# An attention and mixture-of-experts kernel on one core: two casts ahead of an exponential, an output copy one step later, and the first gates spread by TensorE

## The reference

```python
# attention: batch 4, heads 8, seq S=576, head_dim D=64
scores = scale * np.matmul(q, k.transpose(0, 1, 3, 2))
cum = np.cumsum(np.log(np.clip(f, 0.0001, 1.0)), axis=-1)
scores = np.where(causal, -1e9, scores + cum[..., :, None] - cum[..., None, :])
attn = np.exp(scores - scores.max(-1, keepdims=True))
x = matmul(attn / (attn.sum(-1, keepdims=True) + 1e-9), v)   # to (2304 tokens, 512)
# feed-forward, 512 -> 2048 -> 512
h = x @ w_in
g = np.where(h >= 1, h, np.where(h <= -1, 0, (h + 1) ** 2 / 4))
y = g @ w_out
# mixture of 8 experts, the best one for each token
yn = y / (norm(y) + 1e-6);  en = expert_emb / (norm(expert_emb) + 1e-6)
idx = argmax(yn @ en.T / tau)
out = gate * (relu(y @ w1[idx]) @ w2[idx])                  # 512 -> 1024 -> 512
```

## Time and profile before

| | |
|---|---|
| median of 3 runs | 849.34 us (848.88 to 849.74) |
| the profiled execution | 848.67 us |
| its span, first to last instruction | 846.5 us |
| busy in the span: TensorE, its weight loads | 831.4 us (98%), 778.9 us (92%) |
| VectorE, ScalarE, GpSimd | 410.8, 392.9, 353.0 us |
| mean granted TensorE clock | 0.996 |

### The profile page before, as it was taken

One profiled execution on the slowest core, in us unless ns is written; L12 is line 12 of the kernel. 1 busy time (PEld: TensorE's weight loads), 2 busy tenths in 40 slices (PEclk: granted clock), 3 DMA queues, 4 the chain that ended last, 5 costly groups with the idle time before them and its releaser, 6 DMA issues.

```text
span 846.5 us, 13803 instructions
## 1 busy us (share of the span) xinstructions
PE 831.4 (98%) x5018; PEld 778.9 (92%) x5019; DVE 410.8 (49%) x1002; ACT 392.9 (46%) x916; POOL 353.0 (42%) x366
## 2 busy tenths in 40 slices
PE   7999999999999999999999999999999999999996
PEld 5888888889999999999999999999998998998985
DVE  5888888887555454454444444455534110110200
ACT  6777877876665444534544534433332121111121
POOL 5776778856665020211111202074311692010295
PEclk9999999999999999999999999999999999999999
DMA  7577988962000310301211033252222354304041
GB/s 223 189 246 232 288 264 285 291 207 57 29 1 2 102 57 29 104 29 56 75 56 57 1 103 106 75 163 63 76 101 87 120 167 125 87 37 125 26 138 42
DMA packets 70941, 95.62 MB, mean 113 GB/s; under 512 B 7174, under 2 KB 47110, under 8 KB 70864
## 3 DMA queue, kind: packets, MB, share of 16 engines
q1 hardware_dynamic: 62688, 80.33, 31.3%
q10 hardware_dynamic: 6416, 9.59, 3.2%
q0 software_dynamic: 1760, 4.72, 1.5%
HBM read 70.87 MB, written 24.27 MB: 112 GB/s over the span
## 4 chain that ended last, share of the span: by engine, by line
PE 96%; DVE 2%; DMA 1%; issue 1%; ACT 0%; POOL 0%; POOLq 0%; DVEq 0%; SPq 0%; ACTq 0%
PE psum L1523 25%; PE psum L1525 24%; PE psum L1524 24%; PE psum L1494 6%; PE psum L1450 5%; PE psum L1477 5%; PE psum L1455 2%; PE psum L1447 1%; PE psum L1431 1%; DVE pr L1112 1%; PE psum L1606 1%; PE psum L1590 0%; PE psum L1591 0%; DMA c<-cum_d 0%; DVE ptl L1134 0%
## 5 line engine op out<-in xcount | busy, mean ns | idle before, releaser
L1523 PE MATMUL psum<-xh,winh 128*128 128x384 f32 x384 | 129.0, 336 | 0.0
L1523 PE MATMUL psum<-gh,wouth 128*128 128x384 f32 x384 | 128.3, 334 | 0.2 <-issue 0.2
L1525 PE MATMUL psum<-xh,winl 128*128 128x384 f32 x384 | 128.4, 334 | 0.0
L1524 PE MATMUL psum<-xl,winh 128*128 128x384 f32 x384 | 128.3, 334 | 0.0
L1525 PE MATMUL psum<-gh,woutl 128*128 128x384 f32 x384 | 128.3, 334 | 0.0
L1524 PE MATMUL psum<-gl,wouth 128*128 128x384 f32 x384 | 128.3, 334 | 0.0
L898 ACT ACTIVATE hpos<-psum,minus 128x384 f32<-128x384 f32 x96 | 55.9, 582 | 142.3 <-DVE hclip L1160 142.1
L1165 DVE TENSOR_TENSOR g<-hpos,hsq 128x384 f32<-128x384 f32 x96 | 64.5, 672 | 109.2 <-ACT hsq L900 109.2
L691 POOL TENSOR_TENSOR xst<-xst 128x384 f32<-128x384 f32 x24 | 24.7, 1031 | 178.4 <-DMA xst<-rinv_d 178.2
L1270 DVE SCALAR_TENSOR_TENSOR hl<-psum,hh 128x384 fp32r<-128x384 f32 x48 | 26.8, 558 | 139.4 <-ACT hh L954 139.4
L1169 DVE TENSOR_TENSOR gl<-g,gh 128x384 fp32r<-128x384 f32 x96 | 64.1, 668 | 61.0 <-ACT gh L931 61.0
(11 more groups left out here) (233 smaller groups left out, 1871.6 us busy)
## 6 DMA issues: line engine op xcount, KB each, us to landing
praw<-moe_w SPq DMA_DIRECT2D x48, 256.0 KB, 2.8
qraw<-q SPq DMA_DIRECT2D x15, 448.0 KB, 4.5
vraw<-vk SPq DMA_DIRECT2D x16, 320.0 KB, 3.8
xh<-yh_d SPq DMA_DIRECT2D x20, 256.0 KB, 4.2
xl<-yl_d SPq DMA_DIRECT2D x20, 256.0 KB, 4.6
kraw<-k SPq DMA_DIRECT2D x16, 288.0 KB, 3.8
xa_d<-xo SPq DMA_DIRECT2D x16, 288.0 KB, 4.0
xb_d<-xo SPq DMA_DIRECT2D x16, 288.0 KB, 4.5
```

The lines of the kernel that those rows point to most:

```text
L1523: nc.tensor.matmul(psum_at, ah, bh, start=start, stop=False)
L1524: nc.tensor.matmul(psum_at, ah, bl, start=False, stop=False)
L1525: return nc.tensor.matmul(psum_at, al, bh, start=False, stop=stop)
```

## The change

It has five parts.

1. `CASTS_FIRST` becomes (5, 7). At the ScalarE step whose preceding block is 7 the casts `high(p, 4)` and `high(p, 5)` now stand before `exp(n + 2)`, as they did already for block 5.
2. `copy_early(p)` moves from the step of block 8 to that of block 0 of the next pair, behind `high(p, 6)` and `high(p, 7)`.
3. `low(p, 0)` moves one step later, behind the next `masked`.
4. The gates of pair 0: GpSimd makes a 2 x 128 matrix `spread` of ones and zeros; TensorE multiplies it with two rows of `fc` after the warming matmuls, into the banks `PX` and `PY`; ScalarE copies that to `c8`. The two loads for pair 0 go, SP's wait for `cum_out` moves behind four other loads' issues, and GpSimd's zeroing of parts of `pr` also waits for the spread.
5. The embedding's normalization moves from step -4 to 0, its transposes from step 0 to 3, its cast from 1 to 4 and its low part from 2 to 5.

```diff
--- before.py
+++ after.py
@@ -78,7 +78,7 @@
     POOL_HIGH = 4
     EARLY = 2
-    CASTS_FIRST = 5
+    CASTS_FIRST = (5, 7)
     RAW = 2
@@ -213,6 +213,9 @@
         rsum = sb("rsum", [P, 2, NB], F32, actx)
         rden = sb("rden", [P, 2, NB], F32, actx)
+        spread = rturn[0:2, 0, :]
         emb, emb_sq, norm_e = xo[0:E, 1, 0, 0:DM], xo[0:E, 1, 1, 0:DM], xo[0:E, 1, 0, DM:DM + 3]
         fr = pr[0:HEADS, 0:S]
@@ -267,6 +270,7 @@
         f_in = sem("f_in"); clip_ok = sem("clip_ok"); log_ok = sem("log_ok"); cum_ok = sem("cum_ok")
+        spread_ok = sem("spread_ok"); c_spread = sem("c_spread"); c_first = sem("c_first")
         cum_done = sem("cum_done"); cum_out = sem("cum_out")
         passed = sem("passed")
         counts_ok = sem("counts_ok")
@@ -426,8 +430,7 @@
             def load_c(p):
                 if p >= 2:
                     sp.wait_ge(lowest, NB * (p - 1))
-
-                for h in range(2 if p else 1):
+                for h in range(2):
                     sp.dma_start(c8[h * D:(h + 1) * D, p % 2, :],
                                  cum_d[2 * p + h:2 * p + h + 1, :].to_broadcast([D, S])).then_inc(c_in[p % 2], 16)
@@ -468,13 +471,12 @@
             sp.dma_start(tau_sb[:], tau.unsqueeze(0).to_broadcast([P, 1])).then_inc(emb_in, 16)
             sp.wait_ge(cum_ok, 1)
             sp.dma_start(cum_d, fc).then_inc(cum_out, 16)
-            sp.wait_ge(cum_out, 16)
-            load_c(0)
             load_k(1)
             load_v(0)
             sp.dma_start(xst[:].rearrange("p a c -> p (a c)")[:, 0:(NB - RAW) * P],
                          q[1, :, RAW:NB, :].rearrange("p i r -> p (i r)")).then_inc(q1_in, 16)
             load_first(1)
+            sp.wait_ge(cum_out, 16)
             load_c(1)
             load_k(2)
             load_q(2)
@@ -656,7 +658,15 @@
             nc.gpsimd.tensor_copy(mask_b[D:P, :], mask_w[D:P, D:P]).then_inc(const_ok, 1)
             pool.wait_ge(const_ok, 2)
             nc.gpsimd.memset(rinv[:], 0.0).then_inc(zero_ok, 1)
+            nc.gpsimd.memset(spread, 1.0).then_inc(spread_ok, 1)
+            pool.wait_ge(spread_ok, 1)
+            nc.gpsimd.affine_select(out=spread, in_=spread, compare_op=ALU.is_ge, fill=0.0, base=0,
+                                    pattern=[[1, P]], channel_multiplier=-D).then_inc(spread_ok, 1)
+            pool.wait_ge(spread_ok, 2)
+            nc.gpsimd.affine_select(out=spread, in_=spread, compare_op=ALU.is_ge, fill=0.0, base=D - 1,
+                                    pattern=[[-1, P]], channel_multiplier=D).then_inc(spread_ok, 1)
             pool.wait_ge(cum_out, 16)
+            pool.wait_ge(c_spread, 1)
             for i in range(0, NB, 2):
                 x = nc.gpsimd.memset(pr[:, at_tile(i) + keys(i):at_tile(i) + keys(i) + D], 0.0)
             x.then_inc(zero_ok, 1)
@@ -850,8 +860,8 @@
             nc.scalar.copy(kh[:, 0, :], kraw[:]).then_inc(k_h, 1)
             act.wait_ge(q_in, 16)
             nc.scalar.copy(qh[:, 0], qraw[:]).then_inc(q_h, 1)
-            act.wait_ge(cum_out, 16)
-            act.dma_start(c8[D:P, 0, :], cum_d[1:2, :].to_broadcast([D, S])).then_inc(c_in[0], 16)
+            act.wait_ge(c_spread, 1)
+            nc.scalar.copy(c8[:, 0, :].rearrange("p (a c) -> p a c", a=2), psum[:, PX:PY + 1, 0:S // 2]).then_inc(c_first, 1)
             act.wait_ge(esq_ok, 1)
             nc.scalar.activation(norm_e[:, 1:2], norm_e[:, 0:1], ACT.Sqrt).then_inc(eroot_ok, 1)
@@ -902,21 +912,21 @@
             for n in range(-AHEAD, STEPS + 1):
                 p, i = tile_of(n - 1)
-                if i != CASTS_FIRST and 0 <= n + 2 < STEPS:
+                if i not in CASTS_FIRST and 0 <= n + 2 < STEPS:
                     exp(n + 2)
                 if 0 <= n - 1 < STEPS:
                     for k in fills_of(i):
                         high(p, k)
-                if i == CASTS_FIRST and 0 <= n + 2 < STEPS:
+                if i in CASTS_FIRST and 0 <= n + 2 < STEPS:
                     exp(n + 2)
                 p, i = tile_of(n)
-                if i == 8 and 0 <= p < PAIRS:
-                    copy_early(p)
+                if i == 0 and 0 <= p - 1 < PAIRS:
+                    copy_early(p - 1)
                 if p - 1 in X_LOADED and i == 1:
                     split_x(X_LOADED.index(p - 1))
                 if n == STEPS:
                     rise(0)
-                if n == 1:
+                if n == 4:
                     act.wait_ge(en_turned, 1)
                     nc.scalar.copy(ent[:, :, 0:E], psum[:, PY, 0:KD * E].rearrange(
                         "p (k e) -> p k e", e=E)).then_inc(ent_h, 1)
@@ -1092,8 +1102,10 @@
             def masked(n):
                 p, i = tile_of(n)
                 w = keys(i)
-                if i == 0:
-                    dve.wait_ge(c_in[p % 2], 32 * (p // 2 + 1))
+                if n == 0:
+                    dve.wait_ge(c_first, 1)
+                elif i == 0:
+                    dve.wait_ge(c_in[p % 2], 32 * ((p + 1) // 2))
                 if n == 0:
                     dve.wait_ge(zero_ok, 2)
                 dve.wait_ge(scored, n + 1)
@@ -1178,7 +1190,8 @@
                     masked(n + 4)
                 p, i = tile_of(n - 1)
                 if 0 <= n - 1 < STEPS:
-                    for k in fills_of(i):
+                    for k in fills_of(i) if i not in (1, 2) else fills_of(i - 1):
                         low(p, k)
                     if i == 8 and p >= 1:
                         copy_turned(p - 1)
@@ -1207,7 +1220,7 @@
                 if n == STEPS + 4:
                     add(1)
                     low_g(1)
-                if n == -AHEAD:
+                if n == 0:
                     step(nc.vector.reciprocal(tau_inv[:], tau_sb[:]))
                     dve.wait_ge(eroot_ok, 1)
                     step(nc.vector.tensor_scalar_max(norm_e[:, 1:2], norm_e[:, 1:2], 1.0e-30))
@@ -1217,7 +1230,7 @@
                     step(nc.vector.tensor_scalar(norm_e[:, 2:3], norm_e[:, 2:3], 0.5, 1.0e-6, ALU.mult, ALU.add))
                     step(nc.vector.reciprocal(norm_e[:, 1:2], norm_e[:, 2:3]))
                     nc.vector.tensor_scalar(emb, emb, norm_e[:, 1:2], None, ALU.mult).then_inc(en_ok, 1)
-                if n == 2:
+                if n == 5:
                     dve.wait_ge(ent_h, 1)
                     nc.vector.tensor_tensor(ent[:, :, E:2 * E], psum[:, PY, 0:KD * E].rearrange(
                         "p (k e) -> p k e", e=E), ent[:, :, 0:E].bitcast(F32), ALU.subtract).then_inc(ent_ok, 1)
@@ -1419,6 +1432,13 @@
             for n in range(WARM):
                 nc.tensor.matmul(psum[:, PY, :].rearrange("p (a b) -> p a b", a=4), ident_b[:],
                                  ident_b[:].unsqueeze(1).to_broadcast([P, 4, P]), start=True, stop=True)
+            pe.wait_ge(cum_ok, 1)
+            pe.wait_ge(spread_ok, 3)
+            for j in range(2):
+                x = nc.tensor.matmul(psum[:, PX + j, 0:S // 2], spread, fc[0:2, j * (S // 2):(j + 1) * (S // 2)],
+                                     start=True, stop=True)
+            x.then_inc(c_spread, 1)
             MASK_LATER = (4,)
@@ -1551,7 +1571,7 @@
                         turn(p, k)
                 if n == STEPS - 1:
                     up_block(1)
-                if n == 0:
+                if n == 3:
                     pe.wait_ge(en_ok, 1)
                     for m in range(KD):
                         x = nc.tensor.transpose(psum[:, PY, m * E:(m + 1) * E], emb[:, m * P:(m + 1) * P],
```

## The result

The changed kernel takes 841.74 us (median of 4 runs, 840.90 to 842.73). The kernel before took 849.54 beside it (4 runs, 848.88 to 850.49). The ratio is 0.9908, 95% interval 0.9891 to 0.9925. The profiled execution has a span of 839.7 us against 846.5.

The account below looks back on a forecast made before the run. TensorE was taken to bound attention, with two waits of 7.4 us in the pairs. Gains of 6.8 (waits) and 0.8 (start) less 0.45 (end) made 7.15 us: 842.2 us, range 840 to 846 with rivals.

Parts of the forecast that it names:

- the likeliest case: Whole kernel: two TensorE waits in the pairs mostly go and the start gains; 842.2 us, chance 0.58.
- start: First pair: gates spread by TensorE and embedding moved later bring masked(8) near 18.6 instead of 19.38 us; gain 0.8 us.
- pairs 1 to 14 and the last pair: Attention's pairs: TensorE's waits of 7.4 us go, less 0.3 staying and 0.3 in pair 2; gain 6.8 us.
- end: Last pair: the moved output copy delays ScalarE's chain to the first GpSimd splits, near 208 us; loss 0.45 us.
- (a): Middle pairs: casts before exp(1) start low(4) 0.38 earlier, removing the fifth transpose's wait; 0.28 in 13 pairs, 4.3 us in all.
- rival C: Pairs, slower: ScalarE's queue behind the two casts ends later, so turn(0) waits over 0.5 us; about 851 us, chance 0.03.
- (b): Middle pairs: low(0) behind masked(6) removes score(8)'s wait; 0.16 in 10 pairs plus 1.5 in three long stops, 3.1 us.
- (c): Middle pairs: the output's 0.61 us copy moves into ScalarE's 1.14 us wait for masked(4) and costs nothing.
- The holds: Pair 2: GpSimd's instruction holds VectorE's small denominator add; about 1 us of the hold stays, costing 0.3 us.
- the signs that the prediction named as wrong: VectorE L1211 to L1219 over 0.6 us, clock 0.5 after 12 us, L1477 waiting for exp, wait at 208 over 1 us.
- Rival A: Start: GpSimd's splits hold the embedding's VectorE instructions, making the start 1.5 to 3 us worse; 844.5 us, chance 0.22.
- The clock: Start: no TensorE gap, so 2.4 GHz throughout; a fall for some 3.3 us would cost 1.6 us.

Follow-up runs that it names:

- experiment 1: The kernel before with only parts 1 to 3 of the change (casts first, output copy later, low(0) later), old start kept: 842.09 us, ratio 0.9918.
- experiment 3: The changed kernel with part 1 alone taken back, casts 4 and 5 behind exp(1) again: 844.04 us, ratio 0.9951.
- Experiment 4: The changed kernel with part 3 alone taken back, low(0) between masked(5) and masked(6) again: 843.10 us, ratio 0.9938.
- experiment 5: The changed kernel with part 2 alone taken back, the output's copy at the step of block 8 again: 845.27 us, ratio 0.9957.
- experiment 7: The changed kernel with ScalarE's square root moved ahead of its wait for the spread gates: 842.54 us, ratio 0.9923.
- experiment 6: The changed kernel without the denominator's add of 1e-9, the reciprocal taken of the sum itself: 841.17 us, ratio 0.9911.
- Experiment 9: The changed kernel without the denominator's add, with 10 warming matmuls before the spread and 4 after instead of 22 before: 839.37 us, in two groups, ratio 0.9912.
- experiment 2: The changed kernel with parts 1 to 3 taken back, leaving the new start alone: 849.79 us, ratio 1.0008.
- experiment 11: The kernel before, unchanged, in a second single profiled execution: 848.95 us.
- Experiment 8: The kernel before with six more warming matmuls behind score(2), result unused, to fill TensorE's idle gap: 848.81 us, ratio 0.9998.
- experiment 10: The kernel before with only parts 1 to 3 of the change, old start kept, and without the denominator's add: 841.82 us, ratio 0.9915.

## Why the prediction was right, and where its terms were off

**The total and the likeliest case held.** 841.74 against 842.2. By the profiled spans the terms stand like this: start 1.37 measured, 0.8 predicted; pairs 1 to 14 and the last pair together 4.88 + 0.19 + 0.42 = 5.49, 6.8 predicted (the 0.42 is the end's loss, which lies in the last stretch); end -0.42, -0.45 predicted; and 0.3 in the unchanged rest. Two misses of size cancelled in part, which is luck. By medians the steady parts alone won 6.6 us (experiment 1 against the runs of before beside it); the sum without the start had 6.8 - 0.45 = 6.35. The 0.8 of the start has no run behind it.

**Casts first (a): right.** Predicted 0.28 a pair, experiment 3 gives 0.31, with the stop back in the list 13 times. The mechanism, cast to low(4) to the bank of the fifth transpose, is shown by the 0.38 that VectorE idles less and by that experiment. The delayed exponential cost nothing in ordinary pairs, as forecast, so rival C was not met.

**Low(0) behind masked(6) (b): the wait went, but either of two moves removes it.** The prediction credits 0.16 in ten pairs to this move. Experiment 4 leaves it out and the 0.14 doesn't come back; experiment 3 leaves out the earlier casts and keeps this move, and it doesn't come back either. So the mechanism works, and beside (a) it is worth nothing in an ordinary pair. The wait does come back, as 0.40 us and more of idling, in pairs with an x split, where the prediction put 1.5 us in three stops. Taking it back costs 1.4 us of median, at the limit of what the two intervals tell apart.

**The copy one step later (c): mis-sized.** "It costs nothing" was true of its new place within the pairs, but the old place had a price that no sum of mine had: 0.24 a pair and 3.5 us of median (experiment 5). Before, it seems to have lain in the shadow of the wait that (a) removes: with the copy and low(0) moved and the casts late, ordinary pairs take 11.38 for 11.55 (experiment 3), which is little more than low(0)'s 0.14. No run moves the copy alone. Each ordinary pair won 0.48, the forecast was 0.44; it came out because (c), at nothing in the sum, was part of the change.

**The holds: the step that was off by most.** The prediction kept one in pair 2, for 0.3 us beyond its base. Pair 2 was worse than that (11.90, against 11.07 without it), and there were three more in pairs 11 to 13, where GpSimd's split of v, no longer waiting for a late TensorE, begins 0.97, 1.82 and 1.08 us behind the pair's first score in place of 0.33 and falls over the add. The new wait at the transposes for an exponential, 1.7 us in four stops, is one of the signs that the prediction named as wrong; all four lie in pairs 2, 12 and 13.

What they cost together is known less well. From the third to the last pair it is 146.67 to 146.70 us in both executions of the changed kernel and in experiment 7, and 144.83 and 145.75 without the add (experiments 6 and 9): 0.9 to 1.9. Pair 2's share is 0.8. In the others the late gates of pair 12 and the splits of x are mixed in, and experiment 7 has the whole time without their holds.

Both starts can have pair 2's hold. There GpSimd waits for v's transfer. Its split begins 1.58 to 1.68 us behind the pair's first score in the first execution of before, both of the changed kernel and experiments 3 and 7, and the add takes 1.43 to 1.53. It begins at 0.69 and 0.73 in experiments 2 and 4 (new start) and at 2.15 and 2.39 in 11 and 1 (old start), and the add takes 0.35 to 0.60; experiment 5 lies between, at 1.25 and 1.10. So it hangs on the moment at which v lands, measured from the pair's start. Which of the change's parts sets that moment was not isolated.

**The start: order right, value not visible.** Step by step: first score predicted 10.7, measured 10.41; gates 11.4 and 11.15; masked(4) 14.6 and 14.20; masked(8) 18.6 and 18.00; clock 1.00 throughout, as predicted. Rival A was wrong: the seven embedding instructions ran from 12.58 to 14.26 without a hold, the last in 0.47, its length of the earlier trace rows, though GpSimd was splitting nearly all the while. For the last of them that was no hard test: the split before it had only 0.16 us to go, and the next one began 0.24 us into it. Exp(0) starts 1.30 behind the start of the table load; the drain that the Trainium skill (ScalarE: Activation LUTs, What ACT_TABLE_LOAD costs) puts behind such a load did not show.

But the time of experiment 2 says that this start is worth nothing by itself. The traces give three reasons. Experiment 8, which fills the gap and wins nothing either, bears on the first and the third; no run isolates one. First, the base was one execution in which the clock fell; experiment 11 had no fall and started its third pair 0.59 earlier. Its second pair starts at 17.87, and at 17.14 in experiment 1, also with the old start; with the new one it is 17.43 in the changed kernel and 17.94 in experiment 2. Second, the new start hangs on the end of the warming matmuls, and so on when the clock rises: first scores stand at 10.29 to 11.64 us over the eight profiled executions with it and all 22 of them; the old start waited until 11.7 for the gates and hid this. Third, in the old order of the pairs the earlier start was paid back as waits for masked(6) (2.1 us before; 4.0, 3.1 and 4.1 in experiments 2, 8 and 11). There VectorE's split of x, ahead of masked(5), is held by GpSimd to about 0.95 us in seven, five and seven pairs, and was in three before. The prediction had seen these stops but not what makes them long. I did not make an experiment that moves GpSimd's work alone.

**The clock.** In the profiled execution of before it fell, with a mean of 0.996. Of 43 runs of before timed beside the experiments 16 have 0.996 or less, of 41 runs with the new start and its 22 warming matmuls none, and of the 12 with experiment 8's filled gap none. The spans of before are 848.0 to 848.8 at 0.994 and 846.2 to 847.1 at 0.999: by these a fall costs up to 2 us, if the low means are falls. That the new order leaves no such gap was predicted; that it doesn't fall in each execution of before was not (16 of 43, if 0.996 marks a fall), and so its price hardly enters a median. Experiment 9 may show the other side: with 14 warming matmuls instead of 22 two of six runs had 0.994 and took over 7 us more. There is no trace of these two, so the cause stays open; the price of a fall above is far less than 7.

**Which version.** Experiment 9's four faster runs, some 2.8 us under the changed kernel by their medians (838.95), are the best times measured, in part because it leaves out the add, but two of six don't keep them, and its median has an interval of 0.7%. Experiments 6, 10 and 1 (841.17, 841.82, 842.09) can't be told from the changed kernel's 841.74.

## What to carry to other kernels

Cost the old place of a moved instruction too, with the waits that the change removes already gone: what is free in the shadow of one wait is not free afterwards. When the bound engine gets faster, list the pairs of instructions on other engines that exclude each other and ask which of them meet now. And take a start from more than one execution before crediting a time to it, as here the moment at which the clock rose moved the first score by over 1 us.

## What the runs showed of the hardware

The add of 128x9 within SBUF took 0.16 us at the least and, when it met GpSimd's split of v, ran until that ended: 1.53, 1.48, 1.01, 0.93 and 0.81 us. Its usual 0.18 is the same thing: in ten pairs of the changed kernel it meets the last 0.15 us of that split. A reciprocal of 128x9 (all 16, beside GpSimd's instructions of 0.6 to 1.4 us in 15) and the 8x1 instructions kept their 0.20 and 0.14 to 0.26 us. The Trainium skill (SBUF — State Buffer, Who interferes with whom) says that the loser of the shared pair of ports is blocked for the whole instruction; the add agrees: it ended 0.03 us behind GpSimd's instruction in each of the five. The 8x512 multiplication kept its 0.47, but met only the last 0.16 us of a split that began before it; the split that began in it took 1.66 us, 1.57 as a rule. Whether it can be held for a whole instruction, as rival A had it, no run here shows.

The warming matmuls changed from 0.43 to 0.22 us each anywhere between 5.7 and 8.4 us in 13 profiled executions of kernels with the same 22. With the old start TensorE begins nothing new for 1.59 us ahead of 12.02 in the first execution of before, and the granted clock fell near 13.5; it does so for 1.08, 1.10 and 0.71 us in experiments 1, 10 and 11, and there the clock stayed.
